# The third chunk of a quad: q scaled ahead of k, and a turn that waits for k only at its own half

## The reference, cut to what matters

```python
f = 1.0 / (1.0 + np.exp(-f_logit))
for t in range(S):
    state = f[:, :, t, :, None] * state + np.einsum('bhd,bhe->bhde', k[:, :, t], v[:, :, t])
    y[:, :, t] = np.einsum('bhd,bhde->bhe', q[:, :, t], state)
...
for e in range(E):
    h = np.maximum(x @ w1[e], 0.0)
    out += p[:, e:e + 1] * (h @ w2[e])
...
```

## Time and profile before

| what | us |
|---|---|
| median of 3 runs | 1012.02 (1011.11 to 1012.44) |
| the profiled execution's own time | 1011.75 |
| span of its instructions | 1009.7 |
| PE busy | 993.1 |
| DVE busy | 355.3 |
| ACT busy | 285.7 |
| POOL busy | 124.9 |

### The profile page before, as it was taken

How to read it: one execution, slowest core, us unless ns; L and a number is a source line. 1 busy time by engine, 2 the same in 40 slices (tenths; PEclk the granted TensorE clock), 3 DMA queues, 4 the chain that set the end, 5 groups by cost and what they waited for, 6 DMA issues and landing times.

```text
span 1009.7 us, 18104 instructions
## 1 busy us (share of the span) xinstructions
PE 993.1 (98%) x7076; PEld 944.2 (94%) x7076; DVE 355.3 (35%) x778; ACT 285.7 (28%) x607; POOL 124.9 (12%) x147
## 2 busy tenths in 40 slices
PE   8999999999999999999999999999999999999995
PEld 6889999999999999999999999999999999999953
DVE  6555646555543222222222222222222222221443
ACT  5543433343322311111123111111231222222322
POOL 3541221122100500000014000000140000000010
PEclk9999999999999999999999999999999999999998
DMA  9753432532304120000001100000020004111596
GB/s 190 189 101 61 82 71 60 102 66 60 78 13 138 31 96 1 0 0 0 1 1 68 57 0 0 0 0 0 0 106 20 2 1 147 40 62 54 198 339 223
DMA packets 131186, 67.05 MB, mean 66 GB/s; under 512 B 106928, under 2 KB 126896, under 8 KB 131120
## 3 DMA queue, kind: packets, MB, share of 16 engines
q1 hardware_dynamic: 126480, 63.87, 22.9%
q10 hardware_dynamic: 4640, 2.31, 0.8%
HBM read 56.72 MB, written 4.72 MB: 61 GB/s over the span
## 4 chain that ended last, share of the span: by engine, by line
PE 91%; SPq 4%; DVE 2%; DMA 1%; issue 1%; ACT 0%; DVEq 0%; ACTq 0%
PE ph L1721 13%; PE po L1740 13%; PE po L1741 13%; PE po L1742 13%; PE ph L1722 13%; PE ph L1723 13%; PE pair L1669 2%; PE pc L1697 2%; PE pc L1703 1%; PE ph L1963 1%; PE pair L1679 1%; PE po L1979 1%; SPq L766 1%; PE pair L1806 1%; PE pair L1651 1%; PE pair L1655 1%
## 5 line engine op out<-in xcount | busy, mean ns | idle before, releaser
L1317 DVE SCALAR_TENSOR_TENSOR h_lo<-ph,h_hi 128x384 fp32r<-128x384 f32 x256 | 142.7, 558 | 502.4 <-ACT h_hi L1029 501.2
L1029 ACT ACTIVATE h_hi<-ph 128x384 fp32r<-128x384 f32 x256 | 126.0, 492 | 508.1 <-PE ph L1723 508.0
L1721 PE MATMUL ph<-xT,w_hi 128*128 128x384 f32 (+1 forms) x768 | 263.5, 343 | 0.8 <-POOL w_lo L703 0.5
L1740 PE MATMUL po<-w_hi,h_hi 128*128 128x384 f32 x768 | 259.9, 338 | 0.1
L1723 PE MATMUL ph<-xT,w_lo 128*128 128x384 f32 (+1 forms) x768 | 257.1, 335 | 0.0
L1742 PE MATMUL po<-w_hi,h_lo 128*128 128x384 f32 x768 | 257.0, 335 | 0.0
L1722 PE MATMUL ph<-xT,w_hi 128*128 128x384 f32 (+1 forms) x768 | 257.0, 335 | 0.0
L1741 PE MATMUL po<-w_lo,h_hi 128*128 128x384 f32 x768 | 256.8, 334 | 0.0
L1721 PEld LDWEIGHTS ph<-xT,w_hi 128*128 128x128 f32 x768 | 144.2, 188 | 6.4 <-issue 5.2
L1740 PEld LDWEIGHTS po<-w_hi,h_hi 128*128 128x128 f32 x768 | 144.2, 188 | 2.3 <-issue 1.5
L1722 PEld LDWEIGHTS ph<-xT,w_hi 128*128 128x128 f32 x768 | 144.4, 188 | 0.0
(11 more groups left out here) (305 smaller groups left out, 742.5 us busy)
## 6 DMA issues: line engine op xcount, KB each, us to landing
v<-in_moe_w_dram SPq DMA_DIRECT2D x12, 1536.0 KB, 9.8
raw<-in_moe_w_dram SPq DMA_DIRECT2D x6, 1536.0 KB, 8.6
q_in<-in_q_dram SPq DMA_DIRECT2D x48, 96.0 KB, 2.6
v_in<-in_v_dram SPq DMA_DIRECT2D x48, 96.0 KB, 2.6
k_in<-in_k_dram SPq DMA_DIRECT2D x47, 96.0 KB, 2.6
f_in<-in_f_logit_dram SPq DMA_DIRECT2D x43, 96.0 KB, 2.7
v<-in_moe_w_dram SPq DMA_DIRECT2D x6, 576.0 KB, 4.8
x_raw<-yT SPq DMA_DIRECT2D x46, 72.0 KB, 2.2
```

What stands on the lines that cost most here:

```text
L1029: a.activation(h_hi[:, f % 2, :], ph[f % 2][:, 0:BLK], ACT.Relu).then_inc(h_hi_done, 1)
L1317: d.scalar_tensor_tensor(out=h_lo[:, f % 2, :], in0=ph[f % 2][:, 0:BLK], scalar=0.0, in1=h_hi[:, f % 2, :].bitcast(F32), op0=ALU.max, op1= ...
L1721: t.matmul(bank, wh, xh, start=(kk == 0), stop=False, skip_group_check=True)
L1740: t.matmul(bank, hh, w2_hi[:, f, :], start=(f == 0), stop=False, skip_group_check=True)
```

## The change

For part 1 of every quad DVE now scales q first and then takes the maximum and scales k; for part 0 the order stays k, q. The two flag instructions of odd quads move with k, and still end the step. PE's turn no longer waits for `kd_done` ahead of q's transposes, but between q's and k's.

```diff
             def scale_k(m, part):
...
                 d.tensor_tensor(both, both, by_head(k_in, m, part), ALU.mult).then_inc(kd_done, 1)
+                if part == 1 and par == 1:
+                    d.tensor_reduce(top[96:P, 2:3], top[96:P, 0:2], AX.X, ALU.max).then_inc(top_done, 1)
+                    dve.wait_ge(top_done, m // 2 + 1)
+                    d.tensor_scalar(slow_flag[96:P, m // 2:m // 2 + 1], top[96:P, 2:3], SAFE_EXP, None,
+                                    ALU.is_gt).then_inc(flag_done, 1)
...
             def scale_q(m, part):
...
                 d.tensor_tensor(both, both, by_head(q_in, m, part), ALU.mult).then_inc(qd_done, 1)
-                if part == 1 and par == 1:
...
+
+            def scale(m, part):
+
+                if part == 1:
+                    scale_q(m, part)
+                    scale_k(m, part)
+                else:
+                    scale_k(m, part)
+                    scale_q(m, part)
...
             def turn(u):
                 m, i = divmod(u, 2)
                 banks = pair_of(u)
-                pe.wait_ge(kd_done, 2 * (m + 1))
                 pe.wait_ge(qd_done, 2 * (m + 1))
...
                 mm.then_inc(q_turned, 1)
+                pe.wait_ge(kd_done, 2 * (m + 1))
                 for c in range(BT):
```

More of the change, by code:

```diff
@@ L1355, in _ @@
                 elif kind in ("C", "D"):
-                    scale_k(i, int(kind == "D"))
-                    scale_q(i, int(kind == "D"))
+                    scale(i, int(kind == "D"))
                 elif kind == "Z":
-                    scale_k(i, f)
-                    scale_q(i, f)
+                    scale(i, f)
                 elif kind == "k":
```

## The result

The changed kernel takes 1014.24 us (median of 16 runs, 1012.37 to 1016.33), the kernel before in the same series 1012.3 (1011.1 to 1013.15). The ratio is 1.0018 with an interval of 1.0012 to 1.0025: some 1.9 us more, most likely within the 0.2% that I had called the limit, and inside the predicted range. It is 0.4 us above the narrower range that I gave for my own forecast. Two things made it slower, one place in the middle and the opening; the prediction had only the first.

What follows compares the result with a forecast made beforehand. PE, busy 98% of the span, was taken to bound the kernel. Terms 0 (opening) - 0.05 (unit 8) + 1.19 (unit 26) = +1.14 us gave 1013.2 us, range 1011.4 to 1015.0.

Steps and rivals of the forecast that it cites:

- the narrower range that I gave for my own forecast: Whole kernel: 1012.6 to 1013.8 us around the predicted 1013.2 us, chance 0.53.
- Unit 26, +1.19 us: Quad 13: `log_lo` starts ahead of k's product and holds it, so `h_lo` and PE are 1.19 us late.
- Unit 8: Quad 4: q's transposes move ahead of k's product; of 0.35 us only 0.05 counted as gain.
- The branch: At quad 4 q's product starts 0.05 us ahead of POOL's L668, runs at once, and nothing is lost.
- the other branch: At quad 4 q's product starts behind L668, `log_lo` holds k's product: 1.5 us lost, chance 0.2.
- `h_lo` stands behind the whole chain on DVE: Turn of unit 8: PE's piece needs `h_lo`, ending at 67.87, leaving about 0.1 us at most of 0.35.
- Units 14, 16, 22 and 24: Turns where `log_lo` waits for `qd_done`: k's product is ahead by 0.18 us at unit 14, costing nothing.
- The opening, 0 us: Stalls at units 0 and 4: nothing gained or lost, because weight and x transfers cover them.
- A turn that ends earlier only makes that wait longer: After unit 4: PE's 0.34 us wait for x absorbs the earlier turn, so the term is 0.
- a blocked unit 8: Rival: q's product starts behind POOL's L668 at quad 4, 1.5 us more, 1014.7 us; chance 0.2.

Runs made afterwards that it cites:

- experiment 2: The changed kernel with POOL's `log_lo` also waiting for k's product, against the kernel before: 1014.09 us, ratio 1.0009.
- experiment 9: The changed kernel with `log_lo` also waiting for k's product and two constant matmuls ahead of the first hidden matmul, against the kernel before: 1013.08 us, ratio 1.0007.
- experiment 10: The kernel before with the change for quads 4 to 15 alone and `log_lo` also waiting for k's product: 1012.28 us, ratio 1.0000.
- experiment 3: The changed kernel with a short DVE copy ahead of q's product of quad 4, against the kernel before: 1016.24 us, ratio 1.0036.
- experiment 4: The kernel before with the change for quads 0 to 3 alone, the opening: 1013.99 us, ratio 1.0015.
- experiment 12: The kernel before, unchanged except that DVE computes the experts' shares `pn` one piece later: 1011.93 us, ratio 0.9993.
- experiment 1: The kernel before with the change for quad 13 alone: 1013.69 us, ratio 1.0012.
- experiment 7: The kernel before with the change for quads 0 to 3 and two constant matmuls ahead of the first hidden matmul: 1012.54 us, ratio 1.0003.
- experiment 11: The changed kernel with two constant matmuls ahead of the first hidden matmul, `log_lo` as changed, against the kernel before: 1013.64 us, ratio 1.0014.

## Why the prediction was right, and where not

- *Unit 26, +1.19 us.* Shown: 1.19 in the changed kernel, 1.21 with that quad alone, gone in experiments 2, 9 and 10. Each step held: the 0.17 us from q's end to `log_lo` was 0.18, the blocked product ended 0.21 us behind POOL's recorded end where 0.22 was taken, and the `h_lo` behind it passed the loss on in full.
- *Unit 8.* The branch was right: a lead of 0.05 us in the changed kernel, 0.04 in experiment 10, and the other branch when tipped (experiment 3). The size of the term was not. It stood at -0.05 us and measured -0.35, the same in all five traces with the new order and no hold. The step that failed is "`h_lo` stands behind the whole chain on DVE": I took PE's piece to wait for the `h_lo` that ends at 67.87 because it starts just behind it, at 67.98. It starts before the end of that `h_lo` wherever k's product comes last (69.96 against 70.20), so nothing stood in the way of the 0.35 us. q's product started 0.08 us before the recorded end of the instruction in front (68.48 against 68.56), where I had taken 0.09.
- *Units 14, 16, 22 and 24.* k's product came ahead of `log_lo` in all four, by 0.18 or 0.19 us (0.18 reckoned), and took 0.36 us. At unit 14:

```profile
127.79 0.42 DVE L1212 TENSOR_TENSOR qd<-qd,q_in 128x192 f32<-128x192 f32 x1 [0.45 <-ACT qd L981]
...
128.62 0.36 DVE L1199 TENSOR_TENSOR kd<-kd,k_in 128x192 f32<-128x192 f32 x1
...
128.81 1.45 POOL L684 TENSOR_TENSOR log_lo<-f_in,log_hi 128x576 fp32r<-128x576 f32 x1
```

- *The opening, 0 us.* This step failed. "A turn that ends earlier only makes that wait longer" was right as to what happens, and wrong as to its price: I took a longer wait for x as free, since x sets the time. The pieces of 0.53 us ahead of the turn of unit 4 and 0.34 us behind it were joined, and x came 0.93 us later: 1.80 us, of which 1.70 stand in one piece, after which PE ran at 1.2 GHz for 3.4 us. (q's transposes moved up by 0.71 us, from 31.10 to 30.39, and k's by 0.49, from 31.46 to 30.97.) In the four profiled executions of kernels with the opening's change unfilled and unheld (the changed kernel, experiments 2, 3 and 4) that costs 1.5 us each; in the other ten traces, with pieces of 0.99 us and less or with filling, the clock stays at 1.00 and the same stretch takes 7.77 to 7.86 us. Since experiment 12 had 1.51 us of idle time in two pieces without a fall, and the changed kernel 1.79 us around one of 1.70, it is open whether the single piece or the total decides. The part that does not hang on the clock, a later x, the sum did not have either.

In the median the clock carries less than these four traces suggest. A fall like this takes 0.0017 from an execution's mean granted clock, which is recorded to 0.001. Over all executions of the four kernels, 11 of 45 stand at 0.995 or below, of those of the kernel before in the three series 5 of 98. As an estimate, a fall of 1.5 us in a fifth of the executions is some 0.3 us on average. The count is rough: the traced execution of experiment 1 stands at 0.995 without a fall in the opening, and the three filled kernels have 4 of 33, too few to say that filling prevents it. Measured against their own kernels before, the filled medians stand lower than the unfilled ones by 0.74 us (experiment 7 against 4), 0.31 (9 against 2) and 0.52 (11 against the changed kernel), which is in keeping with a cost of this size, but none of the three is clear of noise.

The changed kernel's median is 1.94 us up. With 1.19 for unit 26 and -0.35 for unit 8 this leaves 1.1 us for the opening, and the opening alone measured 1.07 above its own kernel before (experiment 4). The clock would explain less than a third of it. For the rest there is a later first hidden matmul. In the eight traces with the opening's change it comes at 32.72 to 33.81 us, in seven of them at 33.2 or later; in the four with the old opening at 31.71, 32.29, 32.59 and 33.82. That points to a delay by the earlier turns, but chance alone reaches as far, so whether they delay x stays open; it would need many traces of the same kernel. The profiled execution, 4.4 us longer in span, is no guide to the median: 3.2 us of that are there at the turn of unit 31, and the rest comes in the last transfers of the output.

The total was nearer to the forecast than its parts deserve, and that is luck. The sum was 1.14 us, the median 1.94. Unit 26 was right to 0.01 us; unit 8 gave 0.30 us more than its term, and the opening cost 1.1 us where nothing stood; the two errors have opposite signs. The upper part of the range was there for a blocked unit 8 (chance 0.2), and what used it was the opening.

## What to carry to other kernels

When a semaphore is given earlier, look at who waits for it on an engine that can hold up the one that gives it, here POOL and DVE. An instruction of 1.4 us that got in ahead of one of 0.35 us cost 1.19 us, and a lead of 0.05 us decided it elsewhere. A second wait, so that it starts only behind the last short product, took that cost away. Do not take a longer stall for free because something else ends it: earlier work ahead of a late transfer joined two gaps into one of 1.70 us, and TensorE came out of it at half its clock. And an instruction that ends just before another starts need not be what the other waited for; look for a trace in which it ends later.

## What the runs showed of the hardware

- Of a DVE product with both inputs in SBUF and a POOL tensor operation, the one that starts first runs on, down to leads of 0.04 and 0.05 us (unit 8 in experiment 10 and in the changed kernel). POOL's L668 behind q's product took 0.76 us, and 0.59 when it was first. The reduction at 249.13 ran beside `log_lo` at its usual 0.35 us.
- A product of 0.35 us held by `log_lo` lasts 1.37 or 1.38 us in four kernels (the changed one and experiments 1, 3 and 11) and ends 0.21 to 0.22 us behind POOL's recorded end. The Trainium skill ("SBUF — State Buffer", the section on the bandwidth-pool intuition) gives some 115 ns behind the end of the blocking instruction, for a transfer whose descriptors wait for DVE. Carried over to this case, as the prediction did, it would have put the product's end about 0.25 us later, by estimate; the recorded ends here do not agree with that.
- The granted clock fell to 0.50 within 0.5 us after PE took up work again behind idle pieces of 1.70, 1.78, 1.89 and 2.01 us at the end of the opening, and was back at 1.00 after 3.4 us. It did not fall behind pieces of 0.99 us and less at the same place, nor in the three traces with two matmuls of constants in the gap.
